# Two chained MLPs behind a 7-tap convolution on one core: x and output by channel, 16 slots a turn, side taps spread by transfers

## The reference

```python
# x: (4, 4096, 192), weight: (8 heads, 7 taps)
w = softmax(weight, axis=-1)                      # one set of taps per head of 24 channels
x = causal depthwise convolution of x with w      # 7 taps, zero padding in front of each batch
x = x.reshape(16384, 192)
h = x @ w_in;  x = (h * cos(h)) @ w_out           # layer 1 ("A"), d_ff = 2048
h = relu(x @ w2_in);  out = (h * h) @ w2_out      # layer 2 ("B"), d_ff = 2048
```

## Time and profile before

| | us |
|---|---|
| median of 3 runs | 2344.24 |
| lowest, highest | 2343.52, 2344.26 |
| the profiled execution | 2344.38 |
| its span, first to last instruction | 2342.6 |
| TensorE busy in the span | 2296.1 (98%) |
| VectorE busy | 1892.9 (81%) |
| ScalarE busy | 1773.3 (76%) |

### The profile page before, as it was taken

One profiled execution on the slowest core, in us unless ns is written; L12 is line 12 of the kernel. 1 busy time (PEld: TensorE's weight loads), 2 busy tenths in 40 slices (PEclk: granted clock), 3 DMA queues, 4 the chain that ended last, 5 costly groups with the idle time before them and its releaser, 6 DMA issues.

```text
span 2342.6 us, 49150 instructions
## 1 busy us (share of the span) xinstructions
PE 2296.1 (98%) x20352; PEld 2029.7 (87%) x20352; DVE 1892.9 (81%) x2134; ACT 1773.3 (76%) x1875; POOL 0.2 (0%) x4
## 2 busy tenths in 40 slices
PE   5899999999999999999999999999999999999998
PEld 4698998888898888998888998888988888988896
DVE  7888887888877888878888878888878888878862
ACT  5577777877777777777777777777777777777774
POOL 0000000000000000000000000000000000000000
PEclk9899999999999999999999999999999999999998
DMA  4100000000000000000000000000000000000000
GB/s 114 37 5 15 8 13 13 7 13 13 7 13 13 7 13 13 7 13 13 7 13 10 10 13 13 7 13 7 13 13 13 7 13 7 13 13 7 7 8 14
DMA packets 39308, 33.05 MB, mean 14 GB/s; under 512 B 1516, under 2 KB 38508, under 8 KB 39020
## 3 DMA queue, kind: packets, MB, share of 16 engines
q1 hardware_dynamic: 39100, 32.58, 4.8%
q10 hardware_dynamic: 176, 0.00, 0.0%
HBM read 19.99 MB, written 12.58 MB: 14 GB/s over the span
## 4 chain that ended last, share of the span: by engine, by line
PE 95%; DVE 3%; ACT 1%; issue 1%; DMA 0%; SPq 0%; DVEq 0%; ACTq 0%
PE h L357 10%; PE h L359 10%; PE h L361 10%; PE h L363 10%; PE y_A L402 6%; PE y_A L404 5%; PE y_B L402 5%; PE y_B L404 5%; PE y_A L396 5%; PE y_B L396 5%; PE y_B L400 5%; PE y_A L400 4%; PE y_A L398 4%; PE y_B L398 4%; PE h L367 2%; PE h L365 2%
## 5 line engine op out<-in xcount | busy, mean ns | idle before, releaser
L750 DVE TENSOR_TENSOR g_lo<-g,g_hi 128x1024 fp32r<-128x1024 f32 x512 | 625.6, 1222 | 207.4 <-ACT g_hi L624 204.6
L624 ACT ACTIVATE g_hi<-g 128x1024 fp32r<-128x1024 f32 x512 | 538.7, 1052 | 57.4 <-DVE g L745 56.6
L613 ACT ACTIVATE w<-w,quarter 128x1024 f32<-128x1024 f32 x256 | 295.6, 1155 | 286.5 <-DVE w L738 286.5
L357 PE MATMUL h<-x_side_A,up_side_A 64*128 64x512 f32 x1024 | 396.2, 390 | 21.7 <-DVE x_side_A L791 15.5
L396 PE MATMUL y_A<-g_hi,dn_lo_A 64*128 64x512 f32 x1024 | 406.9, 397 | 6.1 <-DVE g_lo L750 5.9
L402 PE MATMUL y_A<-g_hi,dn_side_A 64*128 64x512 f32 x1024 | 405.4, 396 | 0.0
L357 PE MATMUL h<-x_side_B,up_side_B 64*128 64x512 f32 x1024 | 399.2, 394 | 5.9 <-ACT g L605 3.0
L398 PE MATMUL y_A<-g_hi,dn_hi_A 64*128 64x512 f32 x1024 | 402.5, 393 | 0.0
L396 PE MATMUL y_B<-g_hi,dn_lo_B 64*128 64x512 f32 x1024 | 400.9, 391 | 0.4
L402 PE MATMUL y_B<-g_hi,dn_side_B 64*128 64x512 f32 x1024 | 400.3, 391 | 0.0
L398 PE MATMUL y_B<-g_hi,dn_hi_B 64*128 64x512 f32 x1024 | 400.2, 391 | 0.0
(11 more groups left out here) (96 smaller groups left out, 6223.3 us busy)
## 6 DMA issues: line engine op xcount, KB each, us to landing
rows_in<-x SPq DMA_DIRECT2D x32, 384.0 KB, 3.3
out<-late SPq DMA_DIRECT2D x32, 384.0 KB, 2.6
late<-w_out SPq DMA_DIRECT2D x2, 1536.0 KB, 10.4
w<-w_in SPq DMA_DIRECT2D x1, 1024.0 KB, 5.3
stage_in_side<-w_in SPq DMA_DIRECT2D x2, 512.0 KB, 8.2
late<-w_in SPq DMA_DIRECT2D x2, 512.0 KB, 4.5
late<-w_in SPq DMA_DIRECT2D x4, 256.0 KB, 5.5
taps<-weight ACTq DMA_DIRECT2D x4, 0.7 KB
```

What stands on the lines that cost most here:

```text
L357: mm = pe.matmul(dst, up_side[kind][rows, f], xin_side[kind][rows, :], start=rows is top, stop=z)
L613: act.activation(v, v, ACT.Sin, bias=quarter[:, 0:1], scale=-TURN).then_inc(cosine, 1)
L624: act.activation(g_hi[:, r, :, :], g[:, r, :, :], ACT.Copy).then_inc(hi_made[kind], 1)
L750: dve.tensor_tensor(g_lo[:, r, :, :], g[:, r, :, :], g_hi[:, r, :, :].bitcast(F32), ALU.subtract).then_inc(lo_made[kind], 1)
```

## The change

- x reaches the core as 32 tiles already laid out by channel: 128 rows, each with 518 values of a main channel, then 262 values of a side channel. Row r below 64 holds the first 256 tokens of side channel r, row 64 + r the last 256, each with six tokens of history in front. The host only rearranges and pads. The output is written by channel and transposed on the host. The taps come as one table of 128 rows, the down weights in the order in which they are staged.
- X and Y leave the slot list: 16 slots a turn, no identity, no transposes, no tails, no `two_up_and_down`. Every pair slot has an up and a down part.
- The side taps run on all 128 rows with 256 tokens. SP then spreads the result with four transfers inside SBUF to `conv_both`, where both row halves hold all 512 tokens. Both halves get the high part in one copy; the low part of the side channels has a tensor of its own (`x_side_lo`), so that `x_odd` isn't needed.
- Taps stand in slots 2, 2, 4, 4, 5, 10, 10; ScalarE's split of x in slot 11, VectorE's in slot 15. y goes out from `yt` by two stores.
- In the start the loads of layer 1's up weights go without a wait and in two parts; turn -1 has only the taps and splits.

```diff
-SLOTS = [("A", 0), ("A", 1), ("B", 0), ("A", 2), ("B", 1), ("A", 3), ("X", 0), ("B", 2), ("A", 4),
-         ("B", 3), ("B", 4), ("A", 5), ("A", 6), ("A", 7), ("B", 5), ("B", 6), ("Y", 0), ("B", 7)]
+SLOTS = [("A", 0), ("A", 1), ("B", 0), ("A", 2), ("B", 1), ("B", 2), ("A", 3), ("A", 4),
+         ("A", 5), ("A", 6), ("B", 3), ("A", 7), ("B", 4), ("B", 5), ("B", 6), ("B", 7)]
+FIRST_SLOTS = [("B", 0), ("B", 1), ("B", 2), ("A", 0), ("A", 1), ("A", 2), ("A", 3), ("A", 4),
+               ("A", 5), ("A", 6), ("A", 7), ("B", 3), ("B", 4), ("B", 5), ("B", 6), ("B", 7)]
+LAST_SLOTS = [("A", 0), ("B", 0), ("B", 1), ("B", 2), ("B", 3), ("B", 4), ("B", 5), ("B", 6),
+              ("B", 7), ("A", 1), ("A", 2), ("A", 3), ("A", 4), ("A", 5), ("A", 6), ("A", 7)]
-TAP_SLOTS = (6, 7, 9, 9, 10, 14, 15)
-SPLIT_SLOT = 16
+TAP_SLOTS = (2, 2, 4, 4, 5, 10, 10)
+FIRST_TAP_SLOTS = (5, 6, 7, 8, 9, 10, 11)
+SPLIT_SLOT, LOW_SPLIT_SLOT = 11, 15
+Y1_SLOT, Y2_SLOT = 0, 3
+LATE_SLOTS, LATE_LOW_SLOTS = (6, 9, 13), (7, 10, 15)
...
+            def load_x(t):
+                sp.dma_start(xt[:, :], x[t]).then_inc(x_loaded, 16)
+            def spread_side(done):
+                sp.wait_ge(tap_done, done)
+                for rows in (top, low):
+                    sp.dma_start(conv_both[rows, 0:HALF_TOK], conv_side[top, :]).then_inc(side_spread, 16)
+                    sp.dma_start(conv_both[rows, HALF_TOK:TOK], conv_side[low, :]).then_inc(side_spread, 16)
+            def store_y(t):
+                sp.wait_ge(y2_copied, t + 1)
+                sp.dma_start(out_tiles[t, 0:P, :], yt).then_inc(y_stored, 16)
+                sp.wait_ge(y2_summed, t + 1)
+                sp.dma_start(out_tiles[t, P:D, :], yt_side).then_inc(y_stored, 16)
+            load_x(0)
+            load_layer1_up(0, 0, FIRST_PART)
+            load_layer1_up(1, FIRST_PART, F)
+            sp.dma_start(stage_out, w1o.rearrange("p (c d) -> p c d", d=D)).then_inc(late_loaded, 16)
+            spread_side(K)
+            sp.wait_ge(tap_done, 2 * K)
+            load_x(1)
...
+            spread_side(2 * 2 * K)
+            load_x(2)
             sp.wait_ge(late_lo, 6)
             sp.wait_ge(even_made, 2)
-            sp.dma_start(stage_out, w2o.rearrange("(c p) d -> p c d", p=P)).then_inc(late_loaded, 16)
+            sp.dma_start(stage_out, w2o.rearrange("p (c d) -> p c d", d=D)).then_inc(late_loaded, 16)
...
+            with sp.Fori(4, TILES - 2) as i:
+                store_y(sp.snap(i - 2))
+                spread_side((i + 2) * (2 * K))
+                load_x(sp.snap(i + 2))
...
+            def split_x1(turn):
+                if turn.runs("A"):
+                    act.wait_ge(filled["A"], turn.count("A", NP - 1))
+                act.wait_ge(side_spread, (turn.i + 2) * 64)
+                act.activation(xin_side["A"][:, :], conv_both[:, :], ACT.Copy).then_inc(x1_hi, 1)
+                act.wait_ge(tap_done, (turn.i + 2) * (2 * K))
+                act.activation(xin_hi["A"][:, :], conv[:, :], ACT.Copy).then_inc(x1_hi, 1)
...
             def tap_side(turn, k, done):
...
-                dve.scalar_tensor_tensor(out=conv_side[low, :], in0=xt_side[low, k:k + TOK],
-                                         scalar=taps[low, 1, k:k + 1], in1=conv_side[low, :],
+                dve.scalar_tensor_tensor(out=conv_side[:, :], in0=xt_side[:, k:k + HALF_TOK],
+                                         scalar=taps[:, 1, k:k + 1], in1=conv_side[:, :],
                                          op0=ALU.mult, op1=ALU.add).then_inc(tap_done, 1)
```

More of the change, by code:

```diff
@@ L82, in __init__ @@
         self.peeled = isinstance(i, int)
+        self.first = self.peeled and i == -1
     def runs(self, kind, back=0):
@@ L102, in slots, with before @@
         return LAST_SLOTS if self.peeled and self.i - back >= self.tiles else SLOTS
[L104 to L109, removed]
     def earlier(self, s, n):
[L113 to L119, removed]
+        back = -((s - n) // NS)
+        kind, p = self.slots(back)[(s - n) % NS]
+        return back, kind, p, self.runs(kind, back)
+    def before(self, s, n):
         while True:
-            back = -(at // len(seq(0)))
-            kind, p = seq(back)[at % len(seq(0))]
-            if self.runs(kind, back):
+            s -= n
+            back, kind, p, runs = self.earlier(s, 0)
+            if runs:
                 return kind, self.count(kind, p, back)
@@ L329, in _ @@
             UP, DOWN = 4 * PAIR + 1, 5 * PAIR
-            SHORT = 2 * CB
             def up_waits(turn, s, kind, p):
-                freed = turn.before(turn.slots, s, HB)
+                freed = turn.before(s, HB)
                 if freed:
@@ L356, in up_step @@
                 if j == 0:
-                    mm = pe.matmul(dst, up_side[kind][rows, f], xin_side[kind][rows, :], start=rows is top, stop=z)
+                    side = xin_side[kind] if rows is hi_rows[kind] else xin_side_lo
+                    mm = pe.matmul(dst, up_side[kind][rows, f], side[rows, :], start=rows is top, stop=z)
                 if j == 1:
@@ L363, in up_step @@
                     mm = pe.matmul(dst, up_hi[kind][rows, f], xin_hi[kind][rows, :], start=False, stop=z)
[L364 to L367 removed]
+                if j == 4:
+                    side_hi = up_even[rows, p, :] if n == 0 else up_side[kind][rows, f]
+                    mm = pe.matmul(dst, side_hi, xin_side[kind][rows, :], start=False, stop=z)
                 if rows is top and end:
@@ L377, in down_waits @@
                     pe.wait_ge(late_lo, 8)
-                if kind == "B" and p == 0 and turn.runs("Y"):
+                if kind == "B" and p == 0 and turn.runs("O"):
                     pe.wait_ge(y2_copied, turn.i - 1)
@@ L613, in turned_cosine, with high_part @@
                 act.activation(v, v, ACT.Sin, bias=quarter[:, 0:1], scale=-TURN).then_inc(cosine, 1)
-            def high_part(turn, e, kind, p, back):
-                r = turn.ring(e, back) % RING
-                before = Turn(turn.i - back, TILES, turn.i8 - NP * back)
-                freed = before.before(before.pairs, before.ring(e), RING)
+            def high_part(turn, s, kind, p, back):
+                freed = turn.before(s, RING)
                 if freed:
@@ L626, in body @@
             def body(turn):
+                if turn.first:
+                    layer1_hi(0)
                 for s, (kind, p) in enumerate(turn.slots()):
-                    e, back, made, q = turn.earlier(s, 2)
-                    if made in "AB" and turn.runs(made, back):
-                        high_part(turn, e, made, q, back)
-                    _, back, last, q = turn.earlier(s, 1)
-                    if last == "A" and turn.runs("A", back):
-                        turned_cosine(turn, q, back)
@@ L650, in body @@
+                    if runs:
+                        high_part(turn, s - 2, made, q, back)
+                    back, last, q, runs = turn.earlier(s, 1)
+                    if last == "A" and runs:
+                        turned_cosine(turn, q, back)
+                    if s == Y1_SLOT and turn.runs("A", 1):
+                        read_y1(turn)
+                    if s == Y2_SLOT and turn.runs("O"):
+                        read_y2(turn)
                     if turn.runs(kind):
                         read_h(turn, s, kind, p)
-                    if turn.peeled and turn.i == -1 and kind == "X":
-                        layer1_hi(0)
@@ L777, in tap_side @@
                 if k == 0:
-                    dve.tensor_scalar(conv_side[low, :], xt_side[low, 0:TOK], taps[low, 1, 0:1], None,
+                    dve.wait_ge(x_loaded, (turn.i + 2) * 16)
+                    dve.tensor_scalar(conv_side[:, :], xt_side[:, 0:HALF_TOK], taps[:, 1, 0:1], None,
                                       ALU.mult).then_inc(tap_done, 1)
@@ new lines, in body @@
+                taps_at = FIRST_TAP_SLOTS if turn.slots() is FIRST_SLOTS else TAP_SLOTS
+                done = (turn.i + 1) * (2 * K)
+                if turn.first:
+                    for k in range(K):
+                        tap_side(turn, k, k)
+                    for k in range(K):
+                        tap_main(turn, k, K + k)
+                    layer1_up_lo(0)
+                    split_x1(turn)
+                    layer1_up_lo(1)
+                    layer1_down_lo()
+                    return
```

436 lines of the change are left out of this document (136 added, 300 removed).

## The result

The changed kernel takes **2283.75 us** (median of 4 runs, 2282.86 to 2284.51), the kernel before 2343.98 in 4 runs beside it. The ratio is 0.9743, its 95% interval 0.9726 to 0.976: 60.2 us faster. The forecast was 2287.6, with 2281 to 2308 as the range. The profiled execution took 2284.51, its span is 2282.7 with a mean granted clock of 0.994.

A forecast was written before the change was run, and what follows sets the result against it. The prediction took TensorE's matmuls to bound the kernel, if the other engines hand over in time. From 2344.38 us it took 5.0 (start) and 52.2 (loop) and added 0.4 (end): 2287.6 us, range 2281 to 2308.

The forecast's parts named there:

- The transposes go: Loop, end of turn 1 to end of turn 31: 59 slots X and Y vanish at 0.885 us each, 52.2 us gained.
- rival (c): Loop: the transposes were hidden anyway, turns stay at 70.7 us, only the start pays, 2340 us; chance 0.01.
- VectorE's relief: VectorE, each turn: narrower side taps save 1.55 us and edge copies 0.8, worth nothing by itself except in turn 0.
- The spread: Loop, last side tap to ScalarE's split in slot 11: four transfers take 3.9 us, bounds 3.0 and 7.4.
- The 7.4 at the other end: Upper bound of the time from last side tap to spread data, 0.2 + 1.65 + 5.5 us, from 64-row weight loads.
- The margins: Loop hand-overs: 0.8 us to spare for the spread, no stall up to 4.7; 0.5 from A7 to slot 2.
- A7 to B0: Hand-over at the turn's end: B6's low part ends at 8.1 us against 8.62 for slot 2, 0.5 to spare.
- (a): Loop: a small stall each turn because a hand-over is late, 9 to 30 us in all, 2297 to 2318; chance 0.16.
- (b): Loop: spread of 7.4 us replaces the transposes, 2368 us, slower than before from 6.6; cooled clock each turn 2410; chance 0.05.
- The start: Start to turn 1's last read: first spread lands near 16.7, read ends at 154.2 us, 5.0 gained, bounds 1 and 10.
- The end: Turn 31's last fill to span's end: body grows, tail shrinks to 4.2 us, together -0.05, or -0.4 with VectorE's low part.

The follow-up runs named there:

- experiment 1: Kernel before, with all but the last transpose of each row half left out in the loop's 28 turns, slots kept: 2339.54 us, ratio 0.9983.
- experiment 2: Changed kernel without the spread: host puts all side values on both row halves, side taps run on 128 rows of 512 tokens: 2282.28 us, ratio 0.974.
- experiments 4 to 6: Changed kernel with two, four or six small transfers added ahead of the spread in 26 loop turns: 2288.52, 2319.97 and 2355.71 us.
- six-transfer kernel: Changed kernel with six small transfers added ahead of the spread in 26 loop turns: 2355.71 us, ratio 1.0055.
- Experiment 7: Changed kernel with the first spread issued ahead of the 1.5 MB load of layer 1's down weights: 2279.37 us, ratio 0.9733.
- experiment 8: Changed kernel without spread, side taps twice as wide, remaining up weights' high part before x's split, last weights loaded before turn 0's tap wait: 2275.22 us.
- four stalled kernels: Changed kernel with an added VectorE operation in slot 0 (2308.36 us), or two, four or six transfers ahead of the spread (2288.52, 2319.97, 2355.71 us).

## Why the prediction was right, and where its terms were off

**The transposes go: 52.2, measured 53.06.** The step held. The price of a slot was 1.77 a turn by subtraction (70.69 - 68.92) and came out at 1.78 (70.69 - 68.91); over 59 slots the whole stretch gives 0.899 each instead of 0.885, which makes the 0.9 us. I gave two facts about where the time lay, a difference of turns and the matmuls of the earlier trace rows; experiment 1 shows that the difference was the right one to use. My argument against rival (c) was half true: the matmuls of the transposes were in fact hidden (all but 0.15 us a turn), their slots were not.

**VectorE's relief.** Side taps of 480 ns against 0.51 forecast, and worth nothing in the loop, as said; experiment 2 shows it.

**The spread: 3.9, measured 3.90.** That it came out so close is luck, since its parts were off in opposite ways: the issues followed each other at 0.60 on average where I had 0.55, and the landing after the last issue's start was 2.09 instead of 2.0, but the first issue came 0.02 after the last tap instead of 0.2. The page gives 2.1 for 64 KB from issue to landing. The 7.4 at the other end, from the weight loads, was far off; those loads stood behind a larger one. The Trainium skill's rule (SBUF — State Buffer, the DMA setup cost knee) gave an estimate of 2.15 for the last transfer; the trace agrees with 2.1. Its advice, one large transfer instead of small ones, would gain nothing in this loop, since experiment 2 has the same turn without any spread; experiments 4 to 6 show from where it would.

**The margins.** For the spread I had 0.8 us to spare and a stall from 4.7, measured 1.26 to spare and 5.16: the sum of rounded-up terms was too cautious. For A7 to B0 I had 0.5, measured 0.29. So no stall came (a), but the second margin was closer than I knew, and the price that I gave for a stall was too low: a wait of a matmul costs 0.3 us more than its own length.

**Slower than before (b).** The turn would lose its gain of 1.78 at a spread of 5.16 + 1.78 = 6.94, and start and end push the whole kernel's break-even to about 60.2 / 30 + 5.16 = 7.2, where I had 6.6. Of the clock I had said that a stall could cool it, and that each turn would then cost 1.4 us more. The price was right and the "each turn" was not: with a wait of 2.39 us in each of 26 turns the clock fell behind one of them, for 1.42 us, and the span's mean clock was 0.993. The windows around an ordinary wait of the six-transfer kernel:

```profile
1070.00:1074.00 4.00, 1.60 (x16) 1.13 (x14) 2.36 (x2) 3.97 (x5) 0.00 (x0) 1.00 0.00 0
...
1074.00:1078.00 4.00, 4.00 (x38) 3.29 (x36) 1.60 (x2) 3.97 (x5) 0.00 (x0) 1.00 0.00 0
```

The Trainium skill (TensorE: Matmul & The Clock Gate, HAM oscillation) warns of a loop that waits for a transfer in each pass and pays the warm-up each time. Here the trace shows it once in 26 turns with waits of 2.39 us, and not at all with waits of 0.56 (28 turns) and 1.11 (26 turns).

**The start: 5.0, measured 3.75.** This is the term that was mis-sized, and its parts more than the sum. I had the first spread land near 16.7 and VectorE's low part of the up weights 2.8 us earlier. It landed at 19.5, and the first matmul began at 21.5 where I had 18.5. In the changed kernel VectorE's timeline has (answer to the earlier trace rows)

```profile
24.46 1.76 DVE L540 TENSOR_TENSOR up_lo_A<-w,up_hi_A 128x1536 fp32r<-128x1536 f32 x1 [2.96 <-ACT up_hi_A L423]
```

so it is 0.1 earlier instead of 2.8. The queue was the error: I had 4 MB done 13 us after a start at 2, some 310 GB/s. By the transfers' view, 4.7 MB moved from 1.7 to 18.2 us, 284 GB/s, the next x and the spread among them. The taps of turn 0 then ended at 77.2 instead of 76.3, only 0.9 late of the 2.7 us lost, so turn 0 gave back 1.8 that I hadn't counted; that the start missed by no more than 1.25 is this luck. Behind the last tap the chain of spread, split and low parts was 15.0 us long (the split for B0 begins at 92.20) instead of 14.3, because the last weights, issued at 80.34 behind the spread, land at 86.9, and ScalarE waits 3.66 for them. Experiment 7 shows the spread to be on the path; for the last weights experiment 8 shows it only together with its other move.

**The end: -0.4, measured +3.1.** The tail from the last copy of y_B to the last landing was right: 4.26 against 4.2. The body before it was not: it was to grow by 2.8 and shrank by 0.7 (56.37 to 55.69). I had costed what comes in and goes out, but not the stall of before at 2301, though I cited it for its clock. In the kernel before, TensorE's waits after 2224 and its windows behind the first stall and around the second were

```profile
PE h L357 <- issue: 2.9, 1, 2.9
PE h L357 <- ACT g L605: 2.3, 1, 2.3
PE h L431 <- DVE late L824: 1.5, 1, 1.5
```
```profile
2286.00:2288.00 2.00, 2.00 (x13) 1.66 (x11) 0.45 (x1) 0.00 (x0) 0.00 (x0) 0.50 0.00 0
...
2299.00:2303.00 4.00, 1.74 (x16) 1.12 (x12) 0.68 (x1) 2.12 (x4) 0.00 (x0) 1.00 0.00 0
...
2304.00:2308.00 4.00, 4.00 (x24) 3.13 (x22) 1.25 (x2) 3.91 (x5) 0.00 (x0) 0.57 0.00 0
```

and in the changed kernel one wait is left, with a cool stretch behind it and no other before y_B is complete:

```profile
PE h L316 <- issue: 3.7, 1, 3.7
```
```profile
2230.00:2234.00 4.00, 4.00 (x24) 3.71 (x22) 1.71 (x2) 0.00 (x0) 0.00 (x0) 0.57 0.00 0
```

Gone from the body are the wait of 2.3 and the cool stretch behind it, in which steps came 0.43 us apart instead of 0.23, about 1.7 us too much. The first wait grew by 0.8, but the cool stretch behind it got shorter: from the starts of the matmuls it cost about 2.5 us in the kernel before (2285 to 2290.5) and 1.7 in the changed one, 0.8 gained. That makes 4.0 for the 3.5 that were missed. The third wait, 1.5, ends at 2337.39, in the tail that was costed rightly. All this is read from the two traces and not tried: no run brought the stall back, and why it went isn't shown.

So the answer was right by its mechanism, the loop, which is 53 of 60 us; the errors of start (-1.25) and end (+3.5) and loop (+0.9) added up to 3.1 in the span. What failed beside it are two steps: in the start, the time at which the queue lands the first spread (19.5 instead of 16.7), and in the end, a stall of before that was left out of the sum.

## What to carry to other kernels

Price an operation that shares the bound engine by the difference of whole periods with and without its slot, not by its own busy time: the transposes cost 0.15 us a turn, the slots that they broke up 1.63. A new wait off the bound engine is worth nothing or one for one, so work out its threshold, and look at the waits of the weight loads too, since in these kernels a stall showed there before it showed at a matmul. In a start that is bound by loads, issue the small transfer on which the first work waits ahead of the bulk that is needed later: here one line is worth 5 us.

## What the runs showed of the hardware that was not expected

- A stall shows up first at the weight load. With two transfers added, the load waited 0.26 us each turn, no matmul waited, and the turn was 0.15 longer; in all four stalled kernels the turn grew by the load's wait less 0.10 to 0.12.
- The granted clock can fall behind a wait that usually leaves it alone. With six transfers TensorE waited 2.39 us in each of 26 turns, with the same work ahead of it; 25 times the clock stayed at 1.00, once it was 0.64 in the 4 us behind the wait. In the kernel before, a wait of 2.27 us (TensorE busy for 1.74 of the 4 us up to 2303) was followed by 0.57 in 2304 to 2308. What tells these cases apart isn't shown.
- Four transfers of 64 KB inside SBUF, each with 64 rows, are complete 3.9 us after their source is, 2.4 of it issue time on SP, at 0.5 to 0.6 us each. Two added ahead lengthen the spread by 1.39, four by 2.67, six by 3.95: 0.66 to 0.70 us for each, about the 0.64 from one issue to the next, though they carry only 16 KB each. So the time of a transfer added ahead was that of its issue; other sizes weren't tried.
